# Attention on TensorE: products of two key tiles between the two turns of a block of two steps, outputs and projections of k one step later

## The reference

```python
q_bits = (q @ proj > 0); k_bits = (k @ proj > 0)        # 6 bits a token
mask = bucket(q_bits)[:, :, :, None] == bucket(k_bits)[:, :, None, :]
scores = where(mask, q @ k.T / sqrt(64), -1e9)
attn = exp(scores - max(scores)); attn /= sum(attn) + 1e-9
out = attn @ v
```

## Time and profile before

| | |
|---|---|
| median of three runs | 754.57 us |
| the profiled execution | 755.47 us |
| its span, first to last instruction | 753.7 us |
| TensorE busy over the span | 648.7 us, 86% |
| VectorE busy | 434.8 us, 58% |
| ScalarE busy | 351.3 us, 47% |
| GpSimd busy | 306.4 us, 41% |

### The profile page before, as it was taken

The page is one execution under the profiler, slowest core; times in us unless marked ns, Lnnn a source line. Parts: engine busy times, 40 slices in busy tenths (PEclk is TensorE's granted clock), DMA queues, the critical chain, the costliest instruction groups (busy, mean ns, idle before and its releaser), DMA issues. The chain is left out here.

```text
span 753.7 us, 10437 instructions
## 1 busy us (share of the span) xinstructions
PE 648.7 (86%) x3742; PEld 512.6 (68%) x3743; DVE 434.8 (58%) x705; ACT 351.3 (47%) x530; POOL 306.4 (41%) x192
## 2 busy tenths in 40 slices
PE   3999999999999979207999999999487799799998
PEld 1665666656656659107889998899365578578886
DVE  6878787877876421703456544561378985632222
ACT  3676666776667723004345543451245554622100
POOL 5461643716420025262366544560345655733200
PEclk9999999999999985557999999999789999989999
DMA  9105162451624045345676566710442102122311
GB/s 297 54 1 159 59 216 54 164 173 44 217 79 166 1 178 186 83 171 168 222 253 233 199 212 218 259 48 31 147 173 71 56 1 84 42 84 84 111 43 56
DMA packets 50975, 96.09 MB, mean 127 GB/s; under 512 B 16624, under 2 KB 16624, under 8 KB 50928
## 3 DMA queue, kind: packets, MB, share of 16 engines
q1 hardware_dynamic: 48720, 88.38, 34.7%
q0 software_dynamic: 1920, 6.29, 2.4%
q10 hardware_dynamic: 288, 0.79, 0.3%
HBM read 69.23 MB, written 26.21 MB: 127 GB/s over the span
## 5 line engine op out<-in xcount | busy, mean ns | idle before, releaser
L847 POOL TENSOR_TENSOR w_lo<-stage,w_hi 128x1024 fp32r<-128x1024 f32 x28 | 85.1, 3060 | 85.6 <-ACT w_hi L842 85.6
L243 ACT ACTIVATE probs<-scores,bias,scale 128x768 f32<-128x768 f32 x96 | 95.3, 992 | 43.2 <-DVE bias L301 42.9
L294 DVE TENSOR_REDUCE neg_max<-scores 128x1 f32<-128x768 f32 x96 | 91.5, 953 | 19.1 <-PE scores L389 16.9
L235 ACT COPY probs_t<-turned 128x768 f32<-128x768 f32 x96 | 76.3, 795 | 36.4 <-PE turned L398 36.1
L398 PE MATMUL turned<-ident,probs 128*128 128x128 f32 x576 | 80.8, 277 | 9.6 <-ACT probs_t L235 9.6
L398 PEld LDWEIGHTS turned<-ident,probs 128*128 128x128 f32 x576 | 66.0, 142 | 23.3 <-issue 20.0
L936 PE MATMUL up<-xt_hi,w_hi 128*128 128x256 f32 x256 | 73.3, 286 | 2.6 <-DVE xt_lo L889 2.0
L936 PE MATMUL up<-xt_lo,w_hi 128*128 128x256 f32 x256 | 73.1, 286 | 0.0
L936 PE MATMUL up<-xt_hi,w_lo 128*128 128x256 f32 x256 | 73.1, 286 | 0.0
L410 PE MATMUL pv<-probs_t,v_in 128*64 128x384 f32 x384 | 72.3, 498 | 0.8 <-DVE out_t L308 0.8
L389 PE MATMUL scores<-k_aug,q_aug 76*128 76x384 f32 x192 | 60.0, 394 | 11.1 <-ACT probs L243 5.3
(11 more groups left out here) (164 smaller groups left out, 1401.0 us busy)
## 6 DMA issues: line engine op xcount, KB each, us to landing
stage<-in_w SPq DMA_DIRECT2D x64, 512.0 KB, 4.6
wt_raw<-in_w_tok SPq DMA_DIRECT2D x12, 768.0 KB, 4.4
x_slots<-zeros SPq DMA_DIRECT2D x7, 1024.0 KB, 8.6
y_slots<-zeros SPq DMA_DIRECT2D x7, 1024.0 KB, 10.6
q_raw<-in_qT SPq DMA_DIRECT2D x16, 384.0 KB, 5.4
k_raw<-in_kT SPq DMA_DIRECT2D x14, 384.0 KB, 6.3
x_in<-x_slots SPq DMA_DIRECT2D x10, 512.0 KB, 5.0
y_slots<-y_out SPq DMA_DIRECT2D x8, 512.0 KB, 2.8
```

What stands on the lines that cost most here:

```text
L235: nc.scalar.copy(probs_t[j % 2][:, a, :, t % 3 * P:(t % 3 + 1) * P].rearrange("k (b n) q -> k b n q", b=2), turned[:, :, 0:HALF].rearrange ...
L243: nc.scalar.activation(probs[g % 3][:].rearrange("p (b n) -> p b n", b=2), scores[g % 2][:, :, 0:HALF], ACT.Exp, bias=bias[:, pair, a, t:t ...
L294: nc.vector.tensor_reduce(neg_max[:, pair, a, t:t + 1], scores[g % 2][:, :, 0:HALF], AX.XY, ALU.max, negate=True).then_inc(s_neg, 1)
L847: name.tensor_tensor(w_lo[w][:, r, :], stage[:, r, :], w_hi[w][:, r, :].bitcast(F32), ALU.subtract).then_inc(done, 1)
```

## The change

The products of two key tiles move from the end of the odd step to the end of the even step before it, after its turn. Turn-outs move from odd steps to the even steps after them (TURN_LAG 15 to 16), k's projection from step 7 to step 8 of a pair (K_AT), and both stand between the scores and the turn of their step. q's projection stays in step 5, after its turn. VectorE's loop is not edited, but reads TURN_LAG and K_AT, so it normalises a step later, and makes k's signs in steps 8 and 9, of the second head first. The loop has one step more at its end.

```diff
--- before.py
+++ after.py
@@ -33,10 +33,10 @@
 T_LAG = 2
 PV_LAG = 8
 EVICT_LAG = 14
-TURN_LAG = 15
-
-
-Q_AT, K_AT = 5, 7
+TURN_LAG = 16
+
+
+Q_AT, K_AT = 5, 8
 
 
 def attention(nc, ctx, qT, kT, v, proj, x_all, ident, zeros, load_routing, clear):
@@ -425,15 +425,9 @@
             for of_k in range(2):
                 project(0, (a,), of_k, (side, pv)[of_k])
 
-        for g in range(STEPS + TURN_LAG):
+        def on_the_side(g):
+
             pair, n = divmod(g, 12)
-            if g < STEPS:
-                score(g)
-            if 0 <= g - T_LAG < STEPS:
-                turn(g - T_LAG)
-            if 0 <= g - PV_LAG < STEPS and g % 2 == 1:
-                for m in (g - PV_LAG - 1, g - PV_LAG):
-                    products(*divmod(m, 6))
             if pair + 1 < NPAIRS and n in (Q_AT, K_AT):
                 side_free(g)
                 for a in range(2):
@@ -442,6 +436,22 @@
             if g >= TURN_LAG and (g - TURN_LAG) % 6 == 0:
                 side_free(g)
                 turn_out((g - TURN_LAG) // 6)
+
+
+        for g in range(0, STEPS + TURN_LAG, 2):
+            if g < STEPS:
+                score(g)
+            on_the_side(g)
+            if 0 <= g - T_LAG < STEPS:
+                turn(g - T_LAG)
+            for m in (g - PV_LAG, g - PV_LAG + 1):
+                if 0 <= m < STEPS:
+                    products(*divmod(m, 6))
+            if g + 1 < STEPS:
+                score(g + 1)
+            if 0 <= g + 1 - T_LAG < STEPS:
+                turn(g + 1 - T_LAG)
+            on_the_side(g + 1)
 
 
 E = 8
```

## The result

The changed kernel took 759.95 us, the median of six runs (758.26 to 762.27), against 754.67 (752.93 to 756.47): ratio 1.0082, 95% interval 1.0067 to 1.0098. Slower, as forecast, by 5.3 us between the medians where I had 3.1. The profiled execution took 759.79, 4.3 over the one of before; I use it to say where.

The account below looks back on a forecast made before the run. TensorE's queue was taken to bound attention. A pair of 31.92, +0.73, gave six times +4.4; with ends of +0.6, -0.2 and -1.7 that is +3.1 us, 757.7 for the median; own range 756.0 to 759.5, wide range 751.5 to 762.0.

Parts of the forecast that it names:

- (b): Side work inside the turn's wait: block with turn-out 4.82, with projection 5.17; alone saves 1.57 a pair.
- (a): Products moved between the two turns, by themselves: gain nothing; a block without side work stays 4.82.
- (c): Turn-out of step 10 waits 1.53 for VectorE's k signs: block 6.24, 1.42 over 4.82, six times.
- (g): Ends of attention: pair 0 +0.6, pair 7 -0.2, tail -1.7 us.
- (d): First products in step 2 wait 0.88 for pv's eviction, behind step 1's bias held by GpSimd, six times.
- (e): Exponentials: waits of 0.18 to 0.34 are covered; step 4's bias, held by GpSimd, has 0.15 to spare, priced at 0.
- rival 4: Step 4's bias behind GpSimd passes its 0.15; turn and q's projection 0.6 late, six times: +3.9, 761.6, chance 0.15.
- (f): Loads and clears on SP, released a step later at most: cost nothing.
- Rivals 1 to 4: No pv eviction wait, 752.4 (chance 0.12); no signs' wait, 749.2 (0.10); neither, 743.9 (0.05); step 4's bias late, 761.6 (0.15).
- Rival 3: Neither the pv eviction wait in step 2 nor the signs' wait at step 10: -10.7, 743.9, chance 0.05.

Follow-up runs that it names:

- experiment 5: Changed kernel with TURN_LAG 15 and k's projection at step 7, so that only the products are moved: 754.3 us, ratio 1.0003.
- experiment 6: Changed kernel with the products back at the end of the odd step, so that only the side work is moved: 755.83 us, ratio 1.0019.
- Experiment 2: Changed kernel with k's projection back at step 7: 753.75 us, ratio 0.9991.
- experiment 3: Changed kernel with the eviction of pv one step earlier in VectorE's order (EVICT_LAG 13): 755.42 us, ratio 1.0011.
- experiment 7: Changed kernel with bias made by a tensor_scalar in place of a tensor_tensor: 753.55 us, ratio 0.9988.
- experiment 4: Changed kernel with both k's projection back at step 7 and EVICT_LAG 13: 746.95 us, ratio 0.9899.
- experiment 8: Changed kernel with k's projection at step 7, EVICT_LAG 13 and bias by tensor_scalar: 745.49 us, ratio 0.9881.
- experiment 9: Kernel of experiment 8 with each projection cut into one-head halves, each in an even step of its own: 750.27 us, ratio 0.9949.
- experiment 10: Kernel before the change with bias by tensor_scalar alone: 753.91 us, ratio 0.9994.

## Why the prediction came out too small

The direction, both new waits with their places and their counts, and the mechanisms of the gain were right. The time was 757.7; measured 759.95, and 759.03 in the repeat. The forecast's own range of 756.0 to 759.5 holds the repeat and not the first set; the wide one, 751.5 to 762.0, which takes in rivals, holds both. Of the 2.2 us between 757.7 and 759.95, 1.4 are in the trace (4.5 us at the last turn-out against 3.1) and are explained under (b). The other 0.8 no trace shows.

(a) The new cycle is worth nothing by itself: right, a block without side work and without a new wait is 4.82 before and after. What moving the products changes is what lies in the gap (experiment 5 against 6).

(b) The turn-out in the turn's wait: forecast block 4.82, measured 4.82. A projection: forecast 5.17, measured 5.32 and 5.27. **This is the step that failed: the price of the two blocks with a projection, too small.** I took 4.40 + 0.77, with 0.57 from the turn to what follows. But 0.57 is a turn ahead of scores. Ahead of q's projection it is 0.75 (154.38 to 155.13 above), as it is 0.77 ahead of products in the earlier trace rows. Scores ahead of k's projection take 0.87 (160.28 to 161.15) and not 0.81, and the turn behind it 0.81 ahead of products (161.91 to 162.72) and not 0.77. The projection itself is 0.76, as before. The two blocks are 0.15 and 0.10 over the forecast, six pairs make 1.5 us, 1.6 with the 0.02 of (c); the ends came out 0.2 better (g), which leaves the 1.4 between 3.1 and the trace's 4.5. I had the price of a turn ahead of the products in front of me and used it for the products alone. What in TensorE makes the 0.18 no run here shows. That what follows is fp32 isn't enough: the turn-out of experiment 5 is fp32 too, and turn and turn-out take 0.90 together, 0.03 more than apart. Projections and products, unlike it, are 12 and 64 columns wide in the rows and not 128; whether this is the cause was not tested.

(c) The signs of k: forecast wait 1.53 ahead of the turn-out, block 6.24; measured 1.50 (167.85 less 164.16 and 2.19) and 6.26, six times. (The forecast adds 3.65 and 0.06 to 3.72; it is 3.71.) Experiment 2 takes the wait away. My "bounds 0 to 1.8" were wider than they had to be.

(d) The eviction of pv in step 2: forecast 0.88, block 5.70; measured 5.69, six times. Experiments 3 and 7 take it away by two different edits. Bias(1) ended at 146.70 and GpSimd's instruction at 146.67, as the row of before had it, where both ended within 0.01.

(e) Exponentials: bias(4) was held and cost nothing, as forecast, but with more to spare than 0.15:

```profile
152.41 1.75 DVE L301 TENSOR_TENSOR bias<-neg_max,scale 128x1 f32<-128x1 f32 x1
...
155.24 0.80 ACT L235 COPY probs_t<-turned 128x768 f32<-128x768 f32 x1
...
156.70 0.81 PE L398 MATMUL turned<-ident,probs 128*128 128x128 f32 x6
```

The eviction of turn(3) ends at 156.04, 17.80 after scores(11) where I had 18.0, and turn(4) comes at 18.46 where I had 18.3. With the 0.15 that a release takes after such an eviction (145.53 to 145.68 in step 2) that is 0.5 to spare; 0.18 of it comes from the dearer turn ahead of q's projection. So rival 4 was further from happening than the forecast's 0.15 made it look. And I was wrong to take bias(1) and bias(4) for the only ones that matter: experiment 3 shows a wait behind bias(1) and bias(2), 0.36 at scores(4) (0.25 in its block, as the turn behind waits less), that the late products covered, and experiment 6 one of 0.19.

(f) Loads: no wait for them in the pairs.

(g) The ends: forecast +0.6, -0.2, -1.7; measured +0.40, -0.13, -1.74, together 0.2 better.

Rivals 1 to 4 did not happen: the eviction wait, the signs' wait and the time to spare behind bias(4) were all there. (Rival 4's +3.9 is six times 0.65; its text has 0.6, which gives 3.6.) Rival 3's estimate, the change with neither wait, was -10.7, by 6 x 1.57 and the ends; experiments 4 and 8 are what is nearest to it, -7.5 and -8.9, short by the neighbour price of (b), by the 0.25 of scores(4) in experiment 4 and by the 0.09 of scores(10) in experiment 8.

Open: why the first six runs stand 0.9 us above the next five. The traces of both have the same attention period, and their rests differ by 0.4. The two sets overlap (758.26 to 762.27 and 757.82 to 759.53), and so do the intervals of their ratios, so that it may be chance.

## What to carry to other kernels

Where an engine waits a fixed latency between two of its instructions, what is moved into that gap is free as far as it fits (0.42 us here, of the projection's 0.76), but each move also brings forward a wait on a buffer or sets back its release: list, for each moved step, who frees what it writes, and where in that engine's order the freeing stands. Price a moved instruction by its new neighbours, not by its duration: take the start-to-start times of just that succession from the trace. And when two waits are found, mend both before judging either: alone the edits brought 0.80 and 0.63 a pair, together 2.00.

## What the runs showed of the hardware that I had not expected

A turn of six transposes costs 0.57 us from start to start when scores follow, and 0.75 to 0.77 when projections or products follow. Two heads' projections in different columns of the array cost 0.76, one head's alone 0.75 (experiment 9). A tensor_scalar with a per-partition scalar costs 0.21 where the tensor_tensor of the same 128 elements costs 0.16 when free and, held by GpSimd, up to 1.76 (1.44 and 0.67 in the rows above). The slower instruction is the safer choice where the faster one can be held, but its 0.05 is paid where VectorE has no pause: 0.11 a pair in experiment 10, 0.06 in experiment 7.
